# Eight experts' MLPs on one core: first products two units ahead of the second ones, weight loads and weight splits re-ordered

## The reference

```
x   = decay attention(q, k, v, lam)          # 2 batches, 8 heads, 768 tokens, head size 64
logits = x @ w_gate                          # x: 1536 tokens x 512; 8 experts
e = argmax(logits); gate = softmax(logits)[e]
y[t] = gate[t] * (relu(x[t] @ w1[e]) @ w2[e])     # w1: 512 x 1024, w2: 1024 x 512 for each expert
h = y @ w_in; g = h - tanh(h); out = g @ w_out    # w_in: 512 x 2048, w_out: 2048 x 512
```

## Time and profile before

| what | value |
| --- | --- |
| median of 3 runs | 547.28 us (545.83 to 549.81) |
| profiled execution, its own time | 540.98 us |
| its span | 539.1 us |
| mean granted clock of TensorE in it, as a share of full speed | 0.981 |
| PE busy | 510.1 us, 95% of the span |
| DVE, POOL, ACT busy | 365.8, 319.8, 257.4 us |

### The profile page before, as it was taken

How to read it: one execution, slowest core, us unless ns; L and a number is a source line. 1 busy time by engine, 2 the same in 40 slices (tenths; PEclk the granted TensorE clock), 3 DMA queues, 4 the chain that set the end, 5 groups by cost and what they waited for, 6 DMA issues and landing times.

```text
span 539.1 us, 10850 instructions
## 1 busy us (share of the span) xinstructions
PE 510.1 (95%) x3948; PEld 453.5 (84%) x3949; DVE 365.8 (68%) x522; ACT 257.4 (48%) x467; POOL 319.8 (59%) x263
## 2 busy tenths in 40 slices
PE   5999659999999999999999999999999999999994
PEld 4999649999999999999878888888888888888883
DVE  7444265865536545456299999979987765997771
ACT  1222315766656656666364545454434343543431
POOL 4867046745544444444289898976855553865553
PEclk9999958999999999999999999999999999999998
DMA  8988325765875666766360000001100000100002
GB/s 317 324 296 308 131 75 161 229 221 184 241 232 196 229 205 206 235 192 226 113 222 1 0 1 0 1 2 39 40 0 1 1 1 0 60 20 1 1 0 78
DMA packets 32409, 64.55 MB, mean 120 GB/s; under 512 B 3696, under 2 KB 7792, under 8 KB 32368
## 3 DMA queue, kind: packets, MB, share of 16 engines
q1 hardware_dynamic: 30448, 57.71, 32.4%
q0 software_dynamic: 1920, 6.29, 3.5%
HBM read 57.69 MB, written 6.29 MB: 119 GB/s over the span
## 4 chain that ended last, share of the span: by engine, by line
PE 90%; DVE 3%; issue 2%; DMA 2%; POOL 1%; ACT 1%; SPq 0%; DVEq 0%; ACTq 0%; POOLq 0%
PE bank L318 27%; PE bank L320 26%; PE bank L319 26%; PE bank L1152 2%; PE bank L1127 2%; PE bank L1138 2%; PE bank L1174 1%; PE bank L1164 1%; PE bank L1181 1%; PE bank L1238 1%; DMA wst<-in_w_dram 1%; POOL out_dram L649 1%; DMA x_sorted<-token_rows,tokid 1%; PE bank L1313 1%; ACT x_h L741 0%
## 5 line engine op out<-in xcount | busy, mean ns | idle before, releaser
L608 POOL TENSOR_TENSOR w_l<-wst,w_h 128x512 fp32r<-128x512 f32 x64 | 85.1, 1330 | 86.4 <-ACT w_h L712 86.3
L657 POOL TENSOR_SCALAR big<-h_sq 128x512 uint8<-128x512 f32 x48 | 80.4, 1674 | 37.3 <-ACT h_sq L796 37.0
L670 POOL TENSOR_TENSOR g_l<-g,g_h 128x512 fp32r<-128x512 f32 x48 | 63.8, 1330 | 45.5 <-ACT g_h L806 45.5
L318 PE MATMUL bank<-wo_h,g_h 128*128 128x512 f32 x192 | 75.4, 392 | 0.0
L320 PE MATMUL bank<-wo_l,g_h 128*128 128x512 f32 x192 | 75.1, 391 | 0.0
L319 PE MATMUL bank<-wo_h,g_l 128*128 128x512 f32 x192 | 74.6, 389 | 0.0
L320 PE MATMUL bank<-x_l,win_h 128*128 128x512 f32 x188 | 74.3, 395 | 0.0
L318 PE MATMUL bank<-xs_h,w_h 128*128 (+1 forms) x256 | 71.6, 280 | 2.6 <-issue 1.4
L318 PE MATMUL bank<-x_h,win_h 128*128 128x512 f32 x188 | 73.9, 393 | 0.0
L319 PE MATMUL bank<-x_h,win_l 128*128 128x512 f32 x188 | 73.7, 392 | 0.0
L318 PE MATMUL bank<-h_h,w_h 128*128 128x232 f32 x256 | 71.2, 278 | 0.5 <-DVE h_l L1017 0.4
(11 more groups left out here) (159 smaller groups left out, 1095.5 us busy)
## 6 DMA issues: line engine op xcount, KB each, us to landing
wst<-in_w_dram SPq DMA_DIRECT2D x128, 256.0 KB, 3.6
qk_in<-in_qk_t_dram SPq DMA_DIRECT2D x12, 512.0 KB, 6.2
kv_in<-in_kv_dram SPq DMA_DIRECT2D x12, 512.0 KB, 6.0
win<-in_w_in_dram SPq DMA_DIRECT2D x8, 512.0 KB, 4.4
wo<-in_w_out_dram SPq DMA_DIRECT2D x8, 512.0 KB, 8.0
token_rows<-x_sb SPq DMA_DIRECT2D x12, 256.0 KB, 3.8
x_sorted<-token_rows,tokid POOLq DMA_INDIRECT x12, 5.0
out_dram<-rows,tokid POOLq DMA_INDIRECT x12, 3.1
```

The lines of the kernel that those rows point to most:

```text
L318: pe.matmul(dst, lh, rh, start=start, stop=False, skip_group_check=True)
L608: pool.tensor_tensor(w2_l[:, j % STG], wst2[:, j % STG], w2_h[:, j % 2].bitcast(F32), ALU.subtract).then_inc(w2l_ready, 1)
L657: pool.tensor_scalar(big[:, f % 2], h_sq[:, f % 2], T * T, None, ALU.is_ge).then_inc(big_ready, 1)
L670: pool.tensor_tensor(g_l[:, f % 2], g[:, f % 2], g_h[:, f % 2].bitcast(F32), ALU.subtract).then_inc(gl_ready, 1)
```

## The change

First products run two units ahead of the second ones: F(0) and F(1) stand ahead of the loop, and step j is F(j+2), transposes, G(j). ACT and DVE make w1's parts of unit j+2 ahead of the relu and the hidden's low part of unit j. The relu waits for the second product of two units earlier. SP issues each w1 two units ahead of the w2 that stands beside it. `LATER` spreads the ten tiles over steps 0 to 5: 2, 2, 1, 2, 2, 1. POOL's list is unchanged, and so are the orders in the loop for crowded experts on PE, ACT and DVE.

```diff
+    W2_LATER = 2
...
-    LATER = [[t for t in range(2, NT) if (t - 2) * (JT - 1) // (NT - 2) == j] for j in range(JT)]
+    LATER = [[t for t in range(2, NT) if (t - 2) * (JT - 2) // (NT - 2) == j] for j in range(JT)]
...
-            def weights(src, j, unit, first):
+            def load_w1(src, j, unit, first=False):
...
+            def load_w2(src, j, unit, first=False):
+
                 if not first or j >= STG:
                     sp.wait_ge(second_done, unit - STG + 1)
...
             def expert_loads(e, first=False):
+
                 for j in range(JT):
-                    weights(bass.ds(e, 1), j, JT * e + j, first)
+                    load_w1(bass.ds(e, 1), j, JT * e + j, first)
+                    if j >= W2_LATER:
+                        load_w2(bass.ds(e, 1), j - W2_LATER, JT * e + j - W2_LATER, first)
+                    elif not first:
+                        load_w2(bass.ds(e - 1, 1), JT + j - W2_LATER, JT * e + j - W2_LATER)
...
+            for j in range(JT - W2_LATER, JT):
+                load_w2(bass.ds(E - 1, 1), j, JT * (E - 1) + j)
...
             def hidden(j, unit):
                 act.wait_ge(first_done, unit + 1)
+                ge(act, second_done, unit - 1)
...
                     unit = JT * e + j
+                    if not (last and j + 2 >= JT):
+                        act.wait_ge(first_done, unit + 1)
+                        w1_high(j + 2, unit + 2, arrived(e, j + 2))
                     hidden(j, unit)
                     if first:
                         scale(LATER[j])
-                    if not (last and j + 2 >= JT):
-                        w1_high(j + 2, unit + 2, arrived(e, j + 2))
                     if not (last and j + 1 >= JT):
                         ge(act, second_done, unit)
                         w2_high(j + 1, unit + 1, arrived(e, j + 1))
...
                     unit = JT * e + j
+                    if not (last and j + 2 >= JT):
+                        w1_low(j + 2, unit + 2)
                     hidden(j, unit)
                     if first:
                         scale(LATER[j])
-                    if not (last and j + 2 >= JT):
-                        w1_low(j + 2, unit + 2)
...
                 for j in range(JT):
-                    if j + 1 < JT:
-                        first_product(off, j + 1, JT * e + j + 1)
+                    if j + 2 < JT:
+                        first_product(off, j + 2, JT * e + j + 2)
                     elif not last:
-                        if first:
-                            pe.wait_ge(xsl_ready, NT)
-                            pe.wait_ge(pad_ready, 2)
-                        first_product(offset(e + 1), 0, JT * e + JT)
+                        if j + 2 == JT:
+                            if first:
+                                pe.wait_ge(xsl_ready, NT)
+                                pe.wait_ge(pad_ready, 2)
+                            off = offset(e + 1)
+                        first_product(off, j + 2 - JT, JT * e + j + 2)
...
             first_product(0, 0, 0)
+            first_product(0, 1, 1)
```

More of the change, by code:

```diff
@@ L517, in _ @@
                     for j in range(JT):
-                        weights(bass.ds(e, 1), j, JT * E + JT * w + j, False)
+                        load_w1(bass.ds(e, 1), j, JT * E + JT * w + j)
+                        load_w2(bass.ds(e, 1), j, JT * E + JT * w + j)
                 sp.wait_ge(second_done, JT * (E + OV))
```

## The result

The changed kernel took a median of 572.32 us (570.11 to 573.28, 4 runs), the kernel before 547.61 us (545.83 to 549.81, 4 runs). The two medians alone give a ratio of 1.045; the ratio from undisturbed runs alone is 1.053, with a 95% interval from 1.048 to 1.058, which would put the kernel before near 543 us and the loss near 29. The profiled executions took 573.28 and 540.98 us: 32.3 us apart, where the medians are 24.7 apart.

What follows compares the result with a forecast made beforehand. PE's order and pauses were taken to bound the experts' stage. Losses of 18.1 us in experts 1 to 7 and 5.8 in expert 0 sum to 23.9, on the median of 547.3 giving 571 us; range 558 to 581.

Steps and rivals of the forecast that it cites:

- Due time of w1's parts: Experts' stage: F wants w1's parts 2.68 us after a G's end, not 5.36, while ACT still rounds w2 first.
- The short pause: Experts' steps: POOL blocks DVE's w1 low part, F 0.18 us late, 0.25 with restart, once in two steps.
- rival 3: Only the long steps pay: DVE isn't blocked when POOL is first, short pauses (13 x 0.25) vanish; 563.6 us; chance 0.10.
- the row: Profile of the kernel before: DVE's blocked w1 low part ended 0.55 us after POOL's w2 low part.
- The output's and the slice's steps: Steps j = 1 and j = 3, seven times each: late w1 low parts cost 1.05 and 1.39 us.
- the end's: Last expert: G(63) follows G(62) at once but waits for POOL's w2 low part; 1.04 us.
- Expert 0: Tile scaling ahead of w1's parts makes steps of 4.70 and 4.10 us; F(10) at 119.9, +5.8 us.
- Transfers for w_in: SP's queue: they now have one w1 and one w2 behind them in turn; 0, at most 1.7 us, once.
- ACT's waits for w1's DMA: ACT: its 9.6 us of these waits go, as w1 is issued sooner, but they were not PE's.
- collision of DVE and POOL: Output's step before the change: POOL's w2 low part stretched DVE's w1 low part to 1.71 us from 0.69.
- The clock: TensorE's granted clock: a fall would show the forecast wrong; it had stayed at 1.00 across the pause ahead of F(8).
- Rival 4: The clock falls in expert 0, 28 us of products double, less 6 of pauses: +22 us, 593; chance 0.04.

Runs made afterwards that it cites:

- e8_before_sp_new: The kernel before with only SP's new order: 542.09 us against 542.19, ratio 0.999.
- e9_before_sp_win: The kernel before with SP's new order and w_in's slice loaded behind unit 5: 547.41 us against 544.78, ratio 1.004.
- the second profile: The kernel before, unchanged, run once more for another profile: 546.59 us (one run), span 543.9.
- e2_three_ahead: The changed kernel with ACT and DVE making w1's parts of unit j+3 in step j, not j+2: 544.94 us against 545.13, ratio 1.003.
- e7_after_sp_old: The changed kernel with SP's old order, w1 and w2 of a unit side by side: 576.62 us against 542.19, ratio 1.069.
- e12_one_ahead_win2: The changed kernel with F one unit ahead on PE (LATER as before), w_in's slice behind unit 2: 550.56 us against 546.01, ratio 1.013.

## Why the prediction was right, and where it wasn't

- *Due time of w1's parts*: right. The run with the parts three ahead takes 27 us off, and PE's order with its LATER accounts for 21.8; the two ratios of each pair give 27 and 22 as well.
- *The short pause*: mechanism right, size low. It was 0.28 to 0.31 us and 0.1 for the restart, 0.39 in place of 0.25, since PE followed DVE's end by 0.25 and not by 0.14. The sum holds twelve of them (rival 3 says 13): 12 x 0.14 = 1.7 us. By the Trainium skill's rule (SBUF — State Buffer, Who interferes with whom), read as a whole instruction after the block, it would have been 0.39 too, but for a wrong reason: DVE's end was 0.54 behind POOL's, as in the row.
- *The output's and the slice's steps*: 1.06 and 1.41 for 1.05 and 1.39; the end's 0.88 and 0.1 for 1.04.
- *Expert 0*: F(3) to F(7) started at 90.78, 95.48, 99.67, 104.37 and 109.07, steps of 4.70 and 4.2 us where 4.70 and 4.10 were worked out; F(10) at 120.26 for 119.9.
- *Transfers for w_in, put at 0 and bound by 1.7 us, once*: the step that failed. SP's wait for the rounding of expert 0's slice now stands ahead of a w2 that was issued before it until then. It cost 6.0 us in the profiled run (5.6 up to F(12), 0.4 of clock behind it): I had followed the bytes behind the slice, not the wait ahead of it.
- *ACT's waits for w1's DMA, said to go but not to be PE's*: they went, but the rest is wrong. Before's steady pauses vanish with SP's order alone (`e8_before_sp_new`), and none stands at their place in `e9_before_sp_win` either. What I read as a collision of DVE and POOL was the last link of a chain that began with a late w1, one ACT instruction ahead of the earlier trace rows:

```profile
159.10 0.62 ACT L708 CAST w_h<-wst 128x512 fp32r<-128x512 f32 x1 [1.23 <-DMA wst<-in_w_dram]
```

- *The clock*: the prediction named its fall as a sign of being wrong, and it came, though only behind the pause of 4.07 us, where it cost nearly 3 us; from F(2) on, pauses of up to 1.35 left it at 1.00. Rival 4 had it over the whole of expert 0.

On the profiled pair the terms add up: 23.9 + 0.4 (F(10)) + 6.0 + 1.7 = 32.0, measured 32.3. So on the pair that it was worked out for, the sum was 8 us short. That 571 met 572.3 is partly luck: I added the sum to a median of before that lies 6.3 us above its profiled run, while the changed kernel's profiled run is its longest. The profiled run of before is at the low end of its spread (539.0 to 549.3 over the later runs), and the second profile shows one thing that others lose: up to F(8) 3.8 of the 4.8 us, from the blocked scaling and the half clock behind it. In the changed kernel's profile the longest such scaling is 1.31 us. That its steps spare it longer ones is not shown: with the same steps of PE, the profile of `e2_three_ahead` has one of 3.06 us and a pause of 2.44 behind it.

Left open: why PE starts 0.25 behind DVE's end in the short pauses and 0.14 in the others. DVE's block alone isn't it: before, PE started 0.14 behind a blocked one, and the changed kernel's F(10) started 0.23 behind one of 0.68 us that wasn't blocked.

## What to carry to other kernels

To run one product further ahead halved the time to its operands' parts here (5.36 to 2.68 us), since they weren't made a unit earlier as well: move producer and consumer together. In an engine's in-order list, look at what stands ahead of the part that became urgent, and take its wait as part of the price; the same holds for a DMA queue, where a wait for something unrelated holds every load behind it. Sum up on a profile, but ask where that profile lies in the spread of the runs.

## What the runs showed of the hardware

- A DVE subtraction that collided with one of POOL's (both read SBUF) ended 0.53 to 0.56 us behind it, for POOL's of 1.29 and of 0.74 us.
- A DVE scaling can be held by several POOL instructions in a row: 4.63 us behind four of them in one run, 1.81 in another, for one of 0.48.
- A pause of PE costs its length and 0.07 to 0.1 us at the restart.
- The granted clock fell to 0.50, the level of 1.2 GHz, behind a pause of 4.07 us, and stood at 1.00 (2.4 GHz) from F(2) on through a pause in every six or so microseconds, the longest of 1.35. Between these the length of the pause alone doesn't tell: the clock fell to 0.50 behind 2.37 us in `e7_after_sp_old`, and stayed at 1.00 behind 2.77 in `e12_one_ahead_win2`.
